# Layer one's router logits in two halves of 64 tokens

## The reference

```python
logits = x @ w_gate                      # 4608 x 512 by 512 x 8
e_idx = np.argmax(logits, axis=1)        # one expert for each token
...
eom = 1.0 / (1.0 + np.exp(-(x @ w_output_gate)))
h = np.maximum(x[mask] @ w1[e], 0.0)     # 512 -> 1024
ye = h @ w2[e]                           # 1024 -> 512
out[mask] = gate_w[mask, None] * eom[mask, e, None] * ye
```

## Time and profile before

| | |
|---|---|
| median of three runs | 1459.35 us |
| the profiled execution | 1466.2 us, its span from first to last instruction 1464.3 us |
| PE busy | 1417.5 us, 97% of the span |
| DVE, ACT, POOL busy | 53%, 40%, 36% |
| mean granted TensorE clock | 0.987 of full speed |
| the router's matmuls (L1768) | 320 records |
| attention stage / layer one / layer two | to about 390 us / to about 945 us / to the end |

### The profile page before, as it was taken

How to read it: one execution, slowest core, us unless ns; L and a number is a source line. 1 busy time by engine, 2 the same in 40 slices (tenths; PEclk the granted TensorE clock), 3 DMA queues, 4 the chain that set the end, 5 groups by cost and what they waited for, 6 DMA issues and landing times. The chain is left out here.

```text
span 1464.3 us, 35053 instructions
## 1 busy us (share of the span) xinstructions
PE 1417.5 (97%) x10894; PEld 1221.9 (83%) x10894; DVE 773.5 (53%) x1412; ACT 588.5 (40%) x1026; POOL 521.1 (36%) x573
## 2 busy tenths in 40 slices
PE   7999999999899999999999999789999999999996
PEld 6999999999778888888888888568888888888884
DVE  4888888898955233253433234556223355335331
ACT  5788878887323121142322123313112233223220
POOL 3445554546542232242333234333222233223221
PEclk9999999999999999999999999899999999999998
DMA  6544444458244111132421112344112343233210
GB/s 135 121 106 111 106 106 107 111 130 220 82 173 147 42 42 41 38 90 92 147 50 37 38 44 100 84 145 152 52 44 86 109 159 131 100 123 127 69 43 28
DMA packets 180854, 141.65 MB, mean 97 GB/s; under 512 B 131131, under 2 KB 149947, under 8 KB 180160
## 3 DMA queue, kind: packets, MB, share of 16 engines
q1 hardware_dynamic: 156976, 92.43, 21.8%
q0 software_dynamic: 19936, 46.42, 10.6%
q10 hardware_dynamic: 3760, 0.33, 0.2%
HBM read 105.92 MB, written 32.67 MB: 95 GB/s over the span
## 5 line engine op out<-in xcount | busy, mean ns | idle before, releaser
L1705 PE MATMUL bank<-wts,xh 128*128 (+1 forms) x640 | 258.6, 404 | 10.3 <-issue 7.2
L855 ACT ACTIVATE hh<-bank 128x512 fp32r<-128x512 f32 x160 | 87.0, 595 | 440.5 <-PE bank L1750 433.1
L1717 PE MATMUL bank<-wts,hh 128*128 (+1 forms) x640 | 259.1, 405 | 2.4 <-DVE hl L1350 2.1
L1706 PE MATMUL bank<-wts,xh 128*128 (+1 forms) x640 | 251.8, 393 | 1.8 <-issue 1.8
L1707 PE MATMUL bank<-wts,xl 128*128 (+1 forms) x640 | 252.6, 395 | 0.8 <-issue 0.8
L1719 PE MATMUL bank<-wts,hl 128*128 (+1 forms) x640 | 251.8, 393 | 0.0
L1718 PE MATMUL bank<-wts,hh 128*128 (+1 forms) x640 | 250.8, 392 | 0.0
L1343 DVE TENSOR_SCALAR ys<-bank,pair 128x512 f32<-128x512 f32 x80 | 60.0, 750 | 283.8 <-PE bank L1719 282.7
L1337 DVE TENSOR_SCALAR hid<-bank 128x512 f32<-128x512 f32 x80 | 55.1, 689 | 202.0 <-PE bank L1707 184.8
L643 POOL DMA_INDIRECT x_tokens<-ys,pair x43 | 43.7, 1016 | 331.9 <-DVE ys L1343 319.4
L643 POOL DMA_INDIRECT out<-ys,pair x43 | 43.6, 1014 | 322.8 <-DVE ys L1343 301.5
(11 more groups left out here) (290 smaller groups left out, 2527.3 us busy)
## 6 DMA issues: line engine op xcount, KB each, us to landing
raw<-in_moe_w SPq DMA_DIRECT2D x52, 1024.0 KB, 9.0
ks<-in_k SPq DMA_DIRECT2D x64, 128.0 KB, 3.0
qs<-in_q SPq DMA_DIRECT2D x64, 128.0 KB, 3.8
vs<-in_v SPq DMA_DIRECT2D x64, 128.0 KB
x_tokens<-xo SPq DMA_DIRECT2D x32, 256.0 KB, 2.7
wts<-raw POOLq DMA_DIRECT2D x4, 1024.0 KB
xin<-x_tokens,pair POOLq DMA_INDIRECT x86
bins<-pair,idx POOLq DMA_INDIRECT x83
```

The costliest lines, as they stand in the source:

```text
L855: eng.activation(hh[:, half * 4:half * 4 + 4, :].rearrange("p a n -> p (a n)"), src[:, :], ACT.Copy).then_inc(s_hh, 1)
L1705: eng.matmul(dst[:, :], xh[:, c, :], wh, start=c == 0, stop=False)
L1706: eng.matmul(dst[:, :], xh[:, c, :], wl, start=False, stop=False)
L1717: eng.matmul(b_y[:, :], hh[:, c, :], wh, start=c == 0, stop=False)
```

## The change

The router's four matmuls become eight. For each 128 features the 128 tokens are split: tokens 0 to 63 are the weights of one matmul, which writes to output lanes 0 to 63, and tokens 64 to 127 those of another, which writes to lanes 64 to 127. The moving side is the same 16 columns for both, and the results lie where they lay. All the rest, waits and the one semaphore increment included, is unchanged.

```diff
                 for c in range(DC):
-                    last = eng.matmul(b_l[:, 0:2 * E], yt[:, c, :], wg2[:, c, :], start=c == 0, stop=c == DC - 1)
+                    for a in range(2):
+                        part = slice(HALF * a, HALF * (a + 1))
+                        last = eng.matmul(b_l[part, 0:2 * E], yt[:, c, part], wg2[:, c, :],
+                                          start=c == 0, stop=c == DC - 1)
                 last.then_inc(s_lg, 1)
```

## The result

The kernel with the change takes 1476.96 us (median of 4 runs, 1475.85 to 1478.42), the kernel before 1459.09 us beside it (1457.96 to 1462.7). The ratio is 1.0114, with a 95% interval of 1.0100 to 1.0128: slower by 17.9 us (14.6 to 18.7 by the interval). The prediction had 1471.9 and a range of 1461 to 1478, with 0.84 on slower.

What follows compares the result with a forecast made beforehand. PE, busy 97% of the span, was taken as the bound, with its sequencer's register load held back by the full router. 32 x 0.27 = 8.6 plus 5 x 0.79 = 3.9 gave 12.5 us, so 1459.35 became 1471.9 us; range 1461 to 1478.

Steps and rivals of the forecast that it cites:

- the prediction's count: PE's sequencer stops when 17 or 18 matmul records ahead have not started, so the load waits for the router's seventh record.
- Into the halves: From L1719's start to the router's first half: 0.32 us instead of 0.23, bounds 0.23 to 0.39.
- To L1750: From L1719's start to the transposes behind the router: 0.32 in, 0.48 for eight pairs, 0.11 out.
- The array alone: From L1719 to L1705 with only the array counted: 1.76 us against 1.86 before, 0.10 us a tile faster.
- A pair of halves: In the router, two halves run side by side; each pair follows the last after 0.06 us, 0.12 for the first two.
- the rival of serial weight loads: Halves with so few columns don't overlap, 0.11 us a pair in the router; 16 us slower, 1475.7 us; chance 0.09.
- The sequencer's term: Per even tile, register load 0.79 us later, slack covers 0.51, so L1705 about 0.27 us later; range 0.18 to 0.38.
- The rest of the layer: Layer one's four branch tiles and the tile after them have no slack and take 0.79 us each: 3.9 us.
- That the sequencer doesn't hold the array: Rival: the queue takes the short records without delaying the load enough; 40 routers give -4 us, 1455.4 us; chance 0.13.
- only part of the delay would be paid: Rival: the sequencer has unseen reserve and half of the 0.27 us is paid; +4 to +6 us, 1464.5 us; chance 0.12.
- the drain at a change of tile shape: Skill rule that a tiling mode change drains the engine, counted into and out of the halves; some 0.09 us a tile.
- The 64-deep window: Skill's issue window; if 64 matmuls, the load would come long before the router and the rival of no sequencer delay would hold.

Runs made afterwards that it cites:

- halves_move2: The change plus the next tile's register loads (need, place, used) read before the router, second run; 1454.48 against 1460.38 us for the kernel before, ratio 0.9958.
- quarters: The change with the router in four parts of 32 tokens, 32 records; 1490.9 against 1466.38 us for the kernel before, ratio 1.0167.
- incs9: The kernel before plus nine semaphore increments on PE's sequencer after the register loads in 32 even tiles; 1485.26 us, ratio 1.0171 to the kernel before.
- one_load: The kernel before plus one unused register load per even tile, absent from the program that ran; ratio 1.0002 to the kernel before.
- mixed_late: The change in the first 34 routers alone, register loads where they were; 1472.52 against 1460.38 us for the kernel before, ratio 1.0083.
- two_loads: The kernel before plus two unused register loads per even tile, absent from the program that ran; ratio 1.0007 to the kernel before.

## Why the prediction was right, and where its sizes were off

**The mechanism.** It was the one forecast: the array gains, the sequencer's register load comes too late, L1705 waits for issue. Taking the load away from behind the router turned +17.9 us into -6 (halves_move2), more and shorter records gave still more (quarters), and adding sequencer work to the kernel before did what the halves do (incs9). What holds the sequencer until the load is another matter: there the prediction's count did not hold, as said below.

**The array's terms.** Into the halves: predicted 0.32 us after L1719, measured 709.88 - 709.56 = 0.32. To L1750: predicted 0.32 + 0.48 + 0.11 = 0.91, measured 0.89. The array alone: predicted 1.76, measured 1.75 where nothing else held it (halves_move2). A pair of halves follows the last after (0.64 - 0.47) / 3 = 0.057 us, from ten records to sixteen in the timelines above, which is the 0.06 I took. Shorter was the start: the first five pairs need 0.47 - 0.21 = 0.26 us, so that the second follows the first after about 0.08 and not 0.12. The halves overlap with 16 columns as well, so the rival of serial weight loads is out.

**The sequencer's term** was forecast at 2.13 us from L1719 to L1705, +0.27, and was 2.13 to 2.25, +0.34 on average. The load was forecast 0.56 us after L1719 and came 0.59 to 0.68 after it over the 32 tiles (read finer than the tenths in the row above). That is close, but not for the reason given, a queue with 17 records in it until the router's seventh has started. By the tile above, some ten had started and about 14 records were ahead; over the 32 tiles it is 12 to 14. The two event waits between the router and the load say more, with the timeline cut off at 709.90 us:

```profile
L1747 PEldq EVENT_SEMAPHORE  x2: 51/51/51, 709.9 to 710.0; - x2
```

```profile
709.88 0.24 PE L1770 MATMUL bank<-wg,yt 128*64 128x16 f32 x2
```

With 17 records ahead the sequencer would have been past the first wait when L1718 started, since L1719 and the router's sixteen are 17. It got there only as the router's first pair started, 0.34 us after L1719, in every one of the 32 tiles. From there two waits and eight transposes took it 0.25 us. In the quarters the same waits come at 700.9 and 701.1, and the timeline cut off at 700.909 us has 11 of the 32 started, so that about 20 were ahead:

```profile
700.80 0.28 PE L1770 MATMUL bank<-wg,yt 128*32 128x16 f32 x11
```

So the sequencer's lead is 17 records with the undivided router, about 14 with the halves and about 20 with the quarters, and not one count. Whether it is the number of short records or the change of tile shape that keeps the sequencer back until the router starts, no run here separates; sixteen records of the undivided shape would. That the forecast count gives nearly the measured time of the load is luck.

**The rest of the layer** was put at 0.79 us for each of five tiles, 3.9 us, and was more. The starts of L1705 at the ends of the stretches, in the timeline of the kernel after:

```profile
418.69 0.50 PE L1705 MATMUL bank<-wts,xh 128*128 x1 [0.36 <-issue]
865.17 0.49 PE L1705 MATMUL bank<-wts,xh 128*128 x1 [0.21 <-issue]
924.79 0.49 PE L1705 MATMUL bank<-wts,xh 128*128 x1 [1.41 <-issue]
959.46 0.79 PE L1705 MATMUL bank<-wts,xh 128*128 x1 [5.96 <-issue]
```

and in that of one_load, which has the instructions of the kernel before (its line L1706 is L1705 there):

```profile
417.59 0.50 PE L1706 MATMUL bank<-wts,xh 128*128 x1
853.25 0.48 PE L1706 MATMUL bank<-wts,xh 128*128 x1
909.16 0.50 PE L1706 MATMUL bank<-wts,xh 128*128 x1
941.14 0.79 PE L1706 MATMUL bank<-wts,xh 128*128 x1 [5.21 <-issue]
```

| stretch | before (one_load) | after | more | predicted |
|---|---|---|---|---|
| 32 even tiles | 435.66 | 446.48 | 10.8 | 8.6 |
| 4 tiles with branches | 55.91 | 59.62 | 3.7 | 3.1 |
| between the layers | 31.98 | 34.67 | 2.7 | 0.8 |
| to the start, and layer two | 933.3 | 934.6 | 1.3 | 0 |
| span | 1456.9 | 1475.4 | 18.5 | 12.5 |

The first three sum to 17.2 us and carry the 17.9 of the medians. The 5 us that the prediction lacks are 2.2 of the mis-sized load and 2.5 of the layer's end. In the tiles with branches the distance from L1719 to L1705 grew by 0.90, 0.80, 0.79 and 1.18 us where 0.79 had been predicted for each; only the last is much off. The rest is in the last two routers. The prediction took 0.79 for the first of them and put the second at 0, since nothing dense follows it. The matmuls behind these two, in the timeline of one_load:

```profile
924.31 0.63 PE L1657 MATMUL bank<-cst,xin 128*128 128x128 f32 x4 [1.34 <-PEq L1815]
933.30 0.63 PE L1759 MATMUL bank<-cst,ys 128*128 128x128 f32 x4 [1.14 <-PEq L1820]
```

and in that of the change:

```profile
940.57 0.69 PE L1657 MATMUL bank<-cst,xin 128*128 128x128 f32 x2 [2.04 <-PEq L1813]
951.54 0.63 PE L1758 MATMUL bank<-cst,ys 128*128 128x128 f32 x4 [2.47 <-PEq L1818]
```

From the last matmul of `second_of` to these it was 3.45 and 2.33 us, and is 4.03 and 3.43. So the second router, put at 0, cost 1.1 us: behind it, too, the array waits for its own sequencer. About 1 us of the 2.7 is left without a place, and its size is unsure: in the first profile of the kernel before the stretch between the layers takes 33.46 us and not 31.98, so that by it only 1.2 us would be the change's. For the 2.7 speaks mixed_late, with the last routers undivided, which has 31.97.

**The profiled execution.** The two profiles shown first, of before and after, differ by only 11 us in span, since the one of before was 7 us slower than its runs' median. Its L1705 at the same four places in the timeline:

```profile
419.56 0.50 PE L1705 MATMUL bank<-wts,xh 128*128 x1 [0.23 <-issue]
855.25 0.48 PE L1705 MATMUL bank<-wts,xh 128*128 x1
911.15 0.50 PE L1705 MATMUL bank<-wts,xh 128*128 x1
944.61 0.79 PE L1705 MATMUL bank<-wts,xh 128*128 x1 [5.44 <-issue]
```

The even tiles (435.69) and the four with branches (55.90) are those of one_load to 0.03 us. The 7.4 us that its span is longer than one_load's lie around them: 2.0 before the first, 1.5 between the layers and 4.0 in layer two. Carrying a difference over to the median, as the prediction did, was right. That its forecast for the span itself, 1476.8 us, is so near to the 1475.4 measured is luck: a slow profile before made up for a cost put too low.

**The rivals.** That the sequencer doesn't hold the array was wrong for the change, and right for halves_move2, where it gave -6 us against the -4 worked out: the even tiles give 3.7 of it (431.93 us against 435.66), and the branch tiles, which had waited for the sequencer before as well, 1.5. That only part of the delay would be paid was wrong too. Of the two rules of the Trainium skill that the prediction weighed, the drain at a change of tile shape (TensorEngine Tiling (Array Packing), Tiling Modes) agrees with 0.32 us into the halves where an undivided router came after 0.23, and costs less than the halves win. The 64-deep window (TensorE: Matmul & The Clock Gate, the section on back-to-back issue) does not show: in layer one 17 matmul records were ahead of the load, 34 with their weight loads, and in the quarters about 20, or 40 with theirs.

## What to carry to other kernels

Where an engine is busy 97% of the time, ask how far its sequencer runs ahead, and over what: here 17 matmul records, which before the split were 2.1 us of the array's work (703.4 to 705.45), and behind the halves 12 to 14 records, which were at most 1.2. Splitting a matmul into more, smaller ones shortens the array's work and with it the time in which the sequencer gets ahead, and register loads, branches or addresses just behind it then come late. So move such instructions ahead of the run of small matmuls first, and split after that: the same halves were 1.1% slower with the loads behind them and 0.4% faster with the loads ahead.

## What the runs showed of the hardware that I had not expected

- A register load whose value isn't used isn't in the program at all (one_load, two_loads), so it can't serve as a delay; an increment of a semaphore is, at about 0.15 us each in a row on PE's sequencer (incs9), where two event waits follow each other after about 0.1.
- One program was level with the kernel before on one chip (0.9999 to 1.0041) and 0.4% faster on another (0.9944 to 0.9971). The one profile of each differs most at one place, where ACT waits for 11.24 us and not for 5.92; that the timed runs differ by the same wait is likely but not shown.
- Sixteen records of 64 columns by 16 take 0.64 us in all, 32 of 32 columns by 16 take 0.45 (after, quarters): four parts side by side go faster still than two. The first part starts 0.31 to 0.32 us after L1719 in both.
- How far PE's sequencer gets ahead is not one count of matmul records: 17 before the undivided router, about 14 in the halves, about 20 in the quarters.
